# Seven products in place of eight for the experts' up projection, with the sums of weight blocks on GpSimd

## The reference

```python
# window attention, 16 heads of 576 tokens: softmax(q k^T / 8 in a window of 64) v  -> x, 1152 x 512
h = x @ w_in                                              # 512 -> 2048
y = (np.maximum(h, 0) + np.log1p(np.exp(-abs(h)))) @ w_out # softplus, 2048 -> 512
p = domain_probs / (domain_probs.sum(-1, keepdims=True) + 1e-09)
for e in range(4):
    out += p[:, e:e+1] * (np.maximum(y @ w1[e], 0) @ w2[e])  # 512 -> 1024 -> 512
```

## Time and profile before

| | |
|---|---|
| median of 3 runs | 655.79 us |
| the profiled execution | 655.72 us |
| its span | 653.9 us |
| PE busy | 644.4 us (99%) |
| DVE, ACT, POOL busy | 289.0, 232.1, 91.2 us |
| HBM | 61 GB/s over the span |
| granted TensorE clock | full (1.0) |

### The profile page before, as it was taken

The page is one execution under the profiler, slowest core; times in us unless marked ns, Lnnn a source line. Parts: engine busy times, 40 slices in busy tenths (PEclk is TensorE's granted clock), DMA queues, the critical chain, the costliest instruction groups (busy, mean ns, idle before and its releaser), DMA issues.

```text
span 653.9 us, 9966 instructions
## 1 busy us (share of the span) xinstructions
PE 644.4 (99%) x3688; PEld 600.6 (92%) x3688; DVE 289.0 (44%) x708; ACT 232.1 (35%) x583; POOL 91.2 (14%) x87
## 2 busy tenths in 40 slices
PE   8999999999999999999999999999999999999998
PEld 7789999999999999999898989898989898989896
DVE  5986764677556575512242412242412252512121
ACT  5887665565445563401131301131301040402020
POOL 1453333233333332000000000000000000000000
PEclk9999999999999999999999999999999999999999
DMA  8914220132000020200030300030400030110101
GB/s 331 352 47 175 75 121 2 33 130 96 1 2 1 33 97 33 98 0 1 0 128 1 130 0 1 0 128 0 128 0 0 0 128 0 64 49 0 48 0 48
DMA packets 11569, 40.56 MB, mean 62 GB/s; under 512 B 2320, under 2 KB 2320, under 8 KB 10256
## 3 DMA queue, kind: packets, MB, share of 16 engines
q1 hardware_dynamic: 11536, 40.13, 17.0%
HBM read 37.77 MB, written 2.36 MB: 61 GB/s over the span
## 4 chain that ended last, share of the span: by engine, by line
PE 95%; DMA 1%; DVE 1%; POOL 1%; ACT 1%; issue 0%; SPq 0%; DVEq 0%
PE ps L720 25%; PE ps L755 20%; PE ps_pT L720 10%; PE ps_score L720 10%; PE ps_score L755 10%; PE ps L740 8%; PE ps_score L740 4%; PE ps_o L740 4%; PE ps_score L681 2%; DMA raw_b<-in_w_out 1%; PE ps_pT L707 1%; PE ps_pT L694 1%; PE ps L762 1%; ACT prob L353 1%; DVE prob L496 0%
## 5 line engine op out<-in xcount | busy, mean ns | idle before, releaser
L442 ACT ACTIVATE hid_hi<-ps 128x384 fp32r<-128x384 f32 x48 | 23.6, 492 | 241.6 <-PE ps L720 241.6
L720 PE MATMUL ps<-xy_hi,wa_hi 128*128 128x384 f32 (+1 forms) x320 | 109.1, 341 | 0.0
L720 PE MATMUL ps<-xy_hi,wa_lo 128*128 128x384 f32 (+1 forms) x320 | 107.3, 335 | 0.0
L720 PE MATMUL ps<-xy_lo,wa_hi 128*128 128x384 f32 (+1 forms) x320 | 107.1, 335 | 0.0
L306 POOL TENSOR_TENSOR sp_c<-sp_e,sp_c 128x384 f32<-128x384 f32 x48 | 64.5, 1344 | 134.7 <-DVE sp_c L512 134.7
L755 PE MATMUL ps<-wb_hi,hid_lo 128*128 128x512 f32 x192 | 74.9, 390 | 0.0
L755 PE MATMUL ps<-wb_lo,hid_hi 128*128 128x512 f32 x192 | 74.9, 390 | 0.0
L755 PE MATMUL ps<-wb_hi,hid_hi 128*128 128x512 f32 x192 | 74.7, 389 | 0.0
L660 DVE SCALAR_TENSOR_TENSOR part<-ps,gate,part 128x512 f32<-128x512 f32 x24 | 18.0, 751 | 104.8 <-PE ps L755 104.8
L720 PEld LDWEIGHTS ps<-xy_hi,wa_hi 128*128 128x128 f32 x320 | 60.1, 188 | 1.4
L720 PEld LDWEIGHTS ps<-xy_lo,wa_hi 128*128 128x128 f32 x320 | 60.1, 188 | 0.4
(11 more groups left out here) (115 smaller groups left out, 1247.5 us busy)
## 6 DMA issues: line engine op xcount, KB each, us to landing
unit_in<-in_units SPq DMA_DIRECT2D x8, 1024.0 KB, 7.0
raw_a<-in_w SPq DMA_DIRECT2D x16, 512.0 KB, 4.2
raw_b<-in_w SPq DMA_DIRECT2D x16, 512.0 KB, 3.8
raw_a<-in_w_in SPq DMA_DIRECT2D x8, 512.0 KB, 5.3
raw_b<-in_w_out SPq DMA_DIRECT2D x8, 512.0 KB, 4.0
out_dram<-part SPq DMA_DIRECT2D x9, 256.0 KB, 2.0
part<-in_units SPq DMA_DIRECT2D x2, 1024.0 KB, 12.3
unit_in<-in_units SPq DMA_DIRECT2D x2, 384.0 KB, 6.5
```

The lines of the kernel that those rows point to most:

```text
L442: act.activation(hid[0][:, f, :], up_banks[f % 4][:, 0:CH], ACT.Relu).then_inc(h_hi, 1)
L720: m = pe.matmul(bank[:, 0:CH], wa[a][:, f, k, :], xy[x][:, bass.ds(c, 1), k, :], start=(k == 0 and i == 0), stop=(k == KT - 1 and i == 2))
```

## The change

The up projection of each expert, Y (1152 tokens x 512) by W (512 x 1024), is computed in blocks of two by two with seven block products in place of eight. The four experts become eight *pairs* q, each one half of an expert's hidden units (512 of them). In a pair the weights are four blocks A11, A12, A21, A22 (each 256 by 256), and the transposed tokens four blocks B11, B12, B21, B22 (256 wide by 576 tokens). With i = 0, 1 for the two tiles of 128 hidden units of a block, PE does fourteen products `(p, i)` in the order of `ORDER`, each 12 matmuls of 288 columns (2 halves of the tokens, 2 tiles of the contracted width, 3 terms), in pairs of PSUM banks Z[i] and Y[i]. The results are put together out of PSUM in part by accumulating several products in one bank, in part by ACT copies and DVE adds (`keep_first`, `keep_second`, `keep_fifth`, `add_c11`, `add_c22`, `add_c12`). The down projection then does all nine tiles of 128 tokens with four tiles f (12 matmuls of 512 columns each), after which DVE adds into `acc`.

The sums and differences of the token blocks (T1 to T4) and their splits are made once: six casts and three sums on ACT and DVE in steps 35 to 47, the rest during the first pair. The sums of the weight blocks (S1 to S4) are made for each of the 16 groups g = 2q + i by four GpSimd operations on 256 columns (`a_sums`), for groups 0 and 1 in steps 40 and 44 of stage 2. ACT and DVE split the seven weight operands (`a_high`, `a_low`), four instructions each for a group. The hardware loops are gone, `acc` is no longer cleared, the tensors have fixed addresses in SBUF, and the PSUM banks are grouped in pairs. The core of the diff:

```diff
+        PRODUCTS = {"P1": (0, "B11"), "P2": (1, "B21"), "P6": (4, "T2"), "P5": (3, "T1"),
+                    "P7": (5, "T3"), "P4": (2, "T4"), "P3": (6, "B22")}
+        ORDER = [("P1", 0), ("P2", 0), ("P1", 1), ("P2", 1)] + [
+            (p, i) for p in ("P6", "P5", "P7", "P4", "P3") for i in range(2)]
...
-            def clear_sums(c):
-
-                pool.wait_ge(y_hi, KT * (c + 1))
-                pool.wait_ge(y_lo, KT * (c + 1))
-                pool.memset(part[:, c, :], 0.0).then_inc(acc_zero, 1)
+            def a_sums(g):
+                a11, a12, a22, a21 = [raw_u[:, g % 2, i, :, :] for i in range(4)]
+                s1, s2, s3, s4 = [asum[:, i, :, :] for i in range(4)]
+                pool.wait_ge(raw_a_in[g % 2], 64 + 16 * (g // 2 + 1))
+                if g > 0:
+                    pool.wait_ge(a_lo, 4 * g)
+                pool.tensor_tensor(s1, a21, a22, ALU.add).then_inc(a_sum, 1)
+                pool.tensor_tensor(s3, a11, a21, ALU.subtract).then_inc(a_sum, 1)
+                pool.wait_ge(a_sum, 4 * g + 1)
+                pool.tensor_tensor(s2, s1, a11, ALU.subtract).then_inc(a_sum, 1)
+                pool.wait_ge(a_sum, 4 * g + 3)
+                pool.tensor_tensor(s4, a12, s2, ALU.subtract).then_inc(a_sum, 1)
...
+                if k in (STEPS - 8, STEPS - 4):
+                    a_sums((k - STEPS + 8) // 4)
+            for g in range(2, 2 * PAIRS):
+                a_sums(g)
...
+            def add_c22(q, i):
+                dve.wait_ge(prod_done, product_count(q, "P7", i))
+                dve.wait_ge(p5_copied, 2 * q + i + 1)
+                dve.tensor_tensor(fifth[i][:, :, :], Z[i], fifth[i][:, :, :], ALU.add).then_inc(c22_added, 1)
...
+            def product(q, p, i):
+                if p == "P1":
+                    pe.wait_ge(a_lo, 4 * (2 * q + i) + 4)
+                if q == 0:
+                    pe.wait_ge(b_lo, READY[PRODUCTS[p][1]])
...
+                elif p == "P1":
+                    pe.wait_ge(out_added, N_TOK * (q - 1) + (5 if i == 0 else 4))
+                elif p == "P2":
+                    pe.wait_ge(out_added, N_TOK * (q - 1) + (7 if i == 0 else 9))
+                if p in ("P6", "P5", "P7", "P4", "P3"):
+                    pe.wait_ge({"P6": p1_copied, "P5": c11_added, "P7": u2_copied,
+                                "P4": c22_added, "P3": p5_copied}[p], 2 * q + i + 1)
+                row, name = PRODUCTS[p]
+                into = (Y if p in ("P2", "P5", "P3") else Z)[i]
+                fresh = p in ("P1", "P2", "P5")
+                for s in range(2):
+                    for k in range(2):
+                        for j, (a, b) in enumerate(TERMS):
+                            m = pe.matmul(into[:, s, :], aop[a][:, i, row, k, :], bop[name][b][:, k, HC * s:HC * s + HC],
+                                          start=(fresh and k == 0 and j == 0), stop=(k == 1 and j == 2),
+                                          skip_group_check=not fresh)
+                m.then_inc(prod_done, 1)
+
+            def down_tokens(q, T):
+                pe.wait_ge(eh_lo, hidden_count(q, "C21" if T < 4 else "C12", 1))
+                if T == 4:
+                    pe.wait_ge(out_added, N_TOK * q + 1)
+                for i, f in enumerate(wb_rows(q)):
...
+            down_width(NB1 * NCH - 1, FT - 3)
+            down_width(NB1 * NCH - 1, FT - 2)
+            for q in range(PAIRS):
+                for p, i in ORDER:
+                    product(q, p, i)
+                    if q == 0 and (p, i) == ("P1", 0):
+                        down_width(NB1 * NCH - 1, FT - 1)
+                for T in range(N_TOK):
+                    down_tokens(q, T)
```

More of the change, by code:

```diff
@@ L61, in two_stage_mlp_after_window_attention @@
+        part = sb("part", 36864, [P, NCH, KT * CH])
         acc = part[:, :, :].rearrange("p c (t n) -> p (c t) n", n=DM)
[L62 to L81, removed]
@@ L438, in _ @@
+                if n == NB1 * NCH - 1:
+                    a_high(f // 4, f % 4)
             hidden_high(NB1 * NCH - 1, FT - 1)
[L440 to L454 removed]
@@ L663, in _ @@
-            expert(0, True, False)
-            with dve.Fori(1, NE - 1) as e:
-                expert(e, False, False)
-            expert(NE - 1, False, True)
+            for i in (7, 8, 9, 10):
+                b_low(i)
+            last = NB1 * NCH - 1
+            first_out(last, 0)
+            first_out(last, 1)
+            first_out(last, 2)
+            late_first()
+            first_out(last, 3)
+            late_second()
+            late_third()
+            b_low(11)
+            b_low(12)
@@ new lines, in _ @@
+            for q in range(PAIRS):
+                add_c11(q, 0)
+                add_c11(q, 1)
+                relu_low(q, "C11", 0)
+                relu_low(q, "C11", 1)
+                if q == 0:
+                    b_low(13)
+                    fourth()
+                    b_low(14)
+                add_c22(q, 0)
+                if q == 0:
+                    b_low(15)
+                add_c22(q, 1)
+                relu_low(q, "C22", 0)
+                relu_low(q, "C22", 1)
+                if q == 0:
+                    pair_down_low(0, 0)
+                    pair_down_low(0, 1)
+                relu_low(q, "C21", 0)
+                relu_low(q, "C21", 1)
+                if q == 0:
+                    pair_down_low(0, 2)
+                    pair_down_low(0, 3)
+                add_c12(q, 0)
+                add_c12(q, 1)
+                relu_low(q, "C12", 0)
+                relu_low(q, "C12", 1)
+                g = 2 * q + 2
+                for T in range(N_TOK):
+                    add_tokens(q, T)
+                    if q + 1 < PAIRS:
+                        if T in (1, 4):
+                            a_low(g + T // 3, 0)
+                            a_low(g + T // 3, 1)
+                        elif T in (2, 5):
+                            a_low(g + T // 3, 2)
+                            a_low(g + T // 3, 3)
+                        elif 6 <= T < N_TOK - 1:
+                            pair_down_low(q + 1, 2 * (T - 6))
+                            pair_down_low(q + 1, 2 * (T - 6) + 1)
@@ new lines, in down_tokens @@
+            def down_tokens(q, T):
[3 more added lines that the diff above has]
+                for i, f in enumerate(wb_rows(q)):
+                    if T == 0:
+                        pe.wait_ge(wb_lo, 16 + 4 * q + i + 1)
+                    for j, (x, a) in enumerate(TERMS):
+                        m = pe.matmul(TOKEN_BANKS[T], ehid[x][:, i, P * T:P * T + P], wb[a][:, f, :],
+                                      start=(i == 0 and j == 0), stop=(i == 3 and j == 2))
+                m.then_inc(tokens_done, 1)
```

409 lines of the change are left out of this document (285 added, 124 removed).

## The result

The changed kernel takes 634.51 us (median of 4 runs, 634.39 to 634.57), the kernel before 655.77 us (4 runs beside it, 655.34 to 655.83). The ratio is 0.9677, with a 95% interval of 0.966 to 0.9694: 3.2% faster. 636.2 us had been forecast, 1.7 more. The profiled execution took 634.55 us, 21.2 less than the 655.72 of before.

A forecast was written before the change was run, and what follows sets the result against it. PE was taken to bound the kernel. From 655.72 us, -20.9 (fewer columns), -0.9 (loops), +0.3 (GpSimd's sums) and +2.0 (first pair) gave 636.2 us, with a range of 633.9 to 642.

The forecast's parts named there:

- What bounds the kernel: PE, busy 99% of the span; fewer or shorter matmuls gain time, other engines' work costs nothing until it comes late.
- Fewer columns, -20.9 us: Experts' up projection: 1344 matmuls of 288 columns replace 1152 of 384, 178.5 us for 199.4, so 20.9 us less.
- the line: Distance between matmul starts against columns, through 384 (0.1731 us) and 512 (0.2268 us); it gives 0.1328 us at 288.
- Rival (3): A weight load holds PE for its recorded 0.19 us, so products take 252.7 us, the kernel 710 us; chance 0.04.
- Loops, -0.9 us: The experts' twelve passes each lose 0.08 us to the hardware loops' jumps; without loops 0.9 us less, between 0 and 1.0.
- Inside a pair, nothing: Pairs 1 to 7, once running: the new handoffs cost PE zero, at most 1 us each.
- the tightest handoff: P7 to P4 in a pair: `add_c22` reads Z[i] while PE does one other product, with 0.55 us to spare.
- Rival (1): Handoffs in a pair don't fit: every P4 waits, 1 us for each of seven pairs, 643.2 us; chance 0.13.
- GpSimd's sums, +0.3 us: Weight sums at steps 40 and 44 of stage 2 make PE wait 0.3 us more, 0 to 1; in pairs nothing.
- Rival (4): GpSimd's sums hold stage 2: at 1.8 us an operation PE waits some 4 us more, 640 us; chance 0.04.
- The first pair, +2.0 us: DVE also makes the token sums in pair 0, so PE waits 2.0 us in all, between 0 and 4.
- the two gaps forecast: Pair 0: PE waits for DVE 0.8 us before the first P4 and 1.0 us before the first token tile.

## Why the prediction was right, and where it was not

**What bounds the kernel.** Right. PE is busy in all of stage 3, and 86 us of new work for VectorE cost PE about half a microsecond (0.39 and 0.12).

**Fewer columns, -20.9 us.** Right: 0.1327 us for the 0.1328 off the line, so 178.4 us for 178.5. That this is the whole mechanism is shown from three sides: the eighth product took it all back (656.27 us), the halves of 144 columns reached the floor of 0.11 us, and no edit to the sums moved a pair. Rival (3), a load that holds PE for 0.19 us, is out. With it goes, for these matmuls, the rule on loads that the prediction quoted from the Trainium skill (page TensorE: Matmul & The Clock Gate, section Part 3: Packing small matmuls): 288 columns came every 0.1327 us, each with a load.

**Loops, -0.9 us.** The amount came, the cause was wrong. Passes and pairs give 22.0 us, 1.1 more than the matmuls' line; but the loops' removal alone gave 0.13 us the other way, within the noise. The excess of 0.07 us a pass sat in the distances themselves, and the products don't have it; why is open. It was what was left over once the matmuls were counted, and got the name of the only other thing there.

**Inside a pair, nothing.** Right, and the slack of the tightest handoff, 0.55 us forecast, was measured at some 0.59. Rival (1) was therefore close by in one sense: two copies more at that place already cost something.

**GpSimd's sums, +0.3 us.** The place was right (step 43), the size 0.12 us. Their real effect was one that the prediction did not read: an operation of VectorE on tensors in SBUF that begins behind the start of a sum takes some 0.53 us longer. It cost the 0.39 us at T2, a place where none was forecast. The first `lost` behind the first group thus came some 1.4 us late, at 224.16 us, and not the 1.0 of the prediction: VectorE's four operations beside the sums were 2.1 us longer in all. The trace of before had the effect already, though in few places. At 37 us, beside `normalise`, and in stage 2:
```profile
37.26 1.07 POOL L299 TENSOR_TENSOR prob<-prob,rinv 128x384 f32<-128x384 f32 x1 [0.59 <-DVE rinv L491]
37.56 1.32 DVE L465 TENSOR_TENSOR wa_lo<-raw_a,wa_hi 128x512 fp32r<-128x512 f32 x1
...
235.13 0.56 DVE L531 TENSOR_TENSOR hid_lo<-sp_l,hid_hi 128x384 fp32r<-128x384 f32 x1
235.16 1.41 POOL L306 TENSOR_TENSOR sp_c<-sp_e,sp_c 128x384 f32<-128x384 f32 x1 [2.51 <-DVE sp_c L512]
```
The first pair has GpSimd ahead, and VectorE takes 1.32 us for what takes 0.69 elsewhere. In the second, VectorE is ahead by 0.03 us and takes its usual 0.56; so it is for 47 of its 48 low parts of the hidden tile, which is why the rows by line look harmless. There it is `lost` that takes 1.41 us in place of 1.26, and its mean of 1.34 in the earlier trace rows is a mixture of the two. Rival (4), twice the time, was forecast at 640 us; forced, it gave 641.1.

**The first pair, +2.0 us: the step that was mis-sized.** It cost 0.39 us, and neither of the two gaps forecast is there. In the timeline of VectorE after:
```profile
262.04 1.42 DVE L788 TENSOR_TENSOR kept<-banks,kept 128x576 f32<-128x576 f32 x2
...
264.95 0.96 DVE L741 TENSOR_TENSOR T_lo<-part,T_hi 128x768 fp32r<-128x768 f32 x1
265.83 1.42 DVE L744 TENSOR_TENSOR tsum<-part,tsum 128x768 f32<-128x768 f32 x2
...
269.76 0.75 DVE L793 TENSOR_TENSOR fifth<-banks,fifth 128x576 f32<-128x576 f32 x1
```
Two operations of 576 columns end 1.42 us after the first one's start; the prediction had 2 x 0.77. One of 768 columns is followed by the next after 0.88 us (264.95 to 265.83), not 0.98. Records of VectorE overlap by some 0.1 us when operations follow each other closely. (The Trainium skill, page Perfetto Trace Analysis, section Optimizing Scalar/DVE Operations, says that the write-acknowledgement part of a profiled operation overlaps with the next instruction; these rows agree, with 0.09 us.) From the first `first_out` to the add ahead of the first P4 are eighteen operations, and the stretch took 14.9 us (255.58 to 270.51) where 16.5 had been forecast. So that add ended 24.2 us after stage 2's last `up` (which ends at 246.35 us in the timeline of PE), not 25.0, though its chain began 0.7 later than forecast, behind the operations that the sums made long; and P4 started at 24.2 + 0.4. The gap at the first token tile went the same way, with ScalarE's part in it: its four splits of w2 took 2.19 us, 0.52 from one to the next, and not 4 x 0.62, so that DVE's last six operations began at 26.6 and not 28.2 us, and DVE made the tile's last operand 0.44 us ahead of PE. The prediction used distances for PE and durations for VectorE and ScalarE, in the same text. With the measured sizes the sum closes: 636.2 - 1.61 (first pair) - 0.18 (step 43) - 0.2 (1.1 in place of 0.9 beside the line) + 0.32 (start of the run) = 634.5 us, against 634.55 of the profiled execution.

## What to carry to other kernels

Where PE is always busy, count the distance between starts of each shape, put a line through two widths that the trace has, and look for the floor that could end it, here the 0.11 us between weight loads. An algorithm with 7/8 of the products pays as long as its smaller tiles stay on that line; here 7 x 0.1327 stood against 6 x 0.1731 for the same work (with 8 x 0.1327 there was no gain at all), and the added work of the others costs only what the tightest handoff has not to spare. Count chains on VectorE by distances too, and if GpSimd is to work beside it, add half a microsecond to each of its operations on SBUF that begin behind one of GpSimd's, and ask what those were on the way to.

## What was not expected of the hardware

- While GpSimd made one sum behind the other, VectorE's operations with all inputs in SBUF took 0.51 to 0.54 us longer whatever their size, if they began behind the start of a sum: 0.56 to 1.07, 0.68 to 1.22, and 0.36 to 0.89 us for one with a single input. GpSimd's own sums went from 0.73 us to 1.05, when they began behind one of VectorE's. An operation of either engine that began first kept its length: 47 low parts of VectorE beside `lost` took 0.56 us as ever. So did, with 0.69 us, six splits in the pairs that began in the last 0.14 us of a sum. An operation on `banks` (PSUM) and one tensor in SBUF was not lengthened (0.54 us, in the run with doubled sums). In the kernel before, beside `normalise` and GpSimd's splits, up to 105 us, fourteen operations of VectorE were lengthened by 0.2 to 0.6 us. (The Trainium skill, page GPSIMD Engine Reference, section 1. Specifications, has its SBUF interfaces "Shared with VectorE (contention with DVE instructions in a 2-port perf mode or with two SBUF inputs)"; the runs agree and put a number on it.)
- Five hardware loops written out changed nothing, neither the distances nor the time (0.9999 [0.999, 1.0008]), though behind the token tiles the first matmuls of 384 columns come 0.18 us apart in either form.
